# Second network: the tensor engine takes its steps in pairs, 18 products with w_in and then 24 with w_out

## The reference

```python
def _attn_ref(q, k, v, alpha):            # 4 x 8 heads, 768 steps, head size 48
    for t in range(S):
        state = alpha[:, :, t, :, None] * state + np.einsum('bhd,bhe->bhde', k[:, :, t], v[:, :, t])
        y[:, :, t] = np.einsum('bhd,bhde->bhe', q[:, :, t], state)

def _moe_ref(x, expert_emb, tau, w1, w2): # 3072 tokens, 384 features, 8 experts of 1024
    for e in range(E):
        mask = expert_idx == e
        h = np.maximum(x[mask] @ w1[e], 0.0)
        out[mask] = gate_w[mask, None] * (h @ w2[e])

def _moe2_ref(x, w_in, w_out):            # 3072 tokens, 384 -> 2048 -> 384
    h = x @ w_in
    g = np.maximum(0.01 * h, h)
    return (g @ w_out).astype(np.float32)
```

## Time and profile before

| what | us |
|---|---|
| median of 3 runs | 819.06 |
| the three runs | 817.20, 819.06, 819.26 |
| span of the profiled execution, first to last instruction | 817.2 |
| second network, first paired place (inner of step 2) to the end | 415.0 to 817.2 |
| PE busy | 801.6 (98% of the span) |
| ACT busy, DVE busy | 346.0, 452.1 |

### The profile page before, as it was taken

One profiled execution on the slowest core, in us unless ns is written; L12 is line 12 of the kernel. 1 busy time (PEld: TensorE's weight loads), 2 busy tenths in 40 slices (PEclk: granted clock), 3 DMA queues, 4 the chain that ended last, 5 costly groups with the idle time before them and its releaser, 6 DMA issues.

```text
span 817.2 us, 17577 instructions
## 1 busy us (share of the span) xinstructions
PE 801.6 (98%) x5259; PEld 719.7 (88%) x5260; DVE 452.1 (55%) x705; ACT 346.0 (42%) x643; POOL 209.0 (26%) x278
## 2 busy tenths in 40 slices
PE   7899999999999999999999999999999999999998
PEld 7788887889989989999889988889998888998987
DVE  7899987686577476566565334433433533433332
ACT  3455554565446256444443333332333333334223
POOL 6567632223343343341241021003003001001000
PEclk9999999999999999999999999999999999999999
DMA  9988762777887887897741110201201001000001
GB/s 222 256 250 248 219 225 85 265 231 278 301 290 250 283 271 225 291 312 228 201 45 21 20 39 1 40 1 39 39 0 39 0 0 39 1 1 20 20 1 39
DMA packets 64130, 108.98 MB, mean 133 GB/s; under 512 B 24199, under 2 KB 45747, under 8 KB 64080
## 3 DMA queue, kind: packets, MB, share of 16 engines
q1 hardware_dynamic: 54896, 93.47, 37.7%
q0 software_dynamic: 5888, 14.85, 5.8%
q10 hardware_dynamic: 3296, 0.06, 0.2%
HBM read 78.89 MB, written 30.85 MB: 134 GB/s over the span
## 4 chain that ended last, share of the span: by engine, by line
PE 90%; DVE 3%; DMA 3%; issue 2%; POOL 1%; ACT 0%; DVEq 0%; ACTq 0%; SPq 0%; POOLq 0%
PE bank L1772 25%; PE bank L1721 24%; PE bank L1694 15%; PE bank L1674 14%; DMA qkas<-qka 2%; PE bank L1516 2%; PE bank L1556 2%; PE bank L1533 2%; PE bank L1564 1%; PE bank L1650 1%; PE bank L1522 1%; PE bank L1576 1%; POOL kt L675 1%; DVE decay L1073 0%; DMA xg<-x_rows,slot_src 0%
## 5 line engine op out<-in xcount | busy, mean ns | idle before, releaser
L1721 PE MATMUL bank<-yT,wts 128*128 128x512 f32 x864 | 217.5, 395 | 0.3 <-DVE yT L1306 0.3
L1772 PE MATMUL bank<-wts,gs 128*128 128x384 f32 x1152 | 215.5, 335 | 0.4 <-ACT os L1023 0.2
L1772 PEld LDWEIGHTS bank<-wts,gs 128*128 128x128 f32 x1152 | 202.0, 188 | 10.9 <-issue 2.0
L1721 PEld LDWEIGHTS bank<-yT,wts 128*128 128x128 f32 x864 | 160.6, 188 | 31.4 <-DVE yT L1306 1.0
L1302 DVE TENSOR_TENSOR g<-bank,small 128x512 f32<-128x512 f32 x96 | 66.4, 691 | 173.9 <-ACT small L929 163.8
L929 ACT ACTIVATE small<-bank 128x512 f32<-128x512 f32 x96 | 57.6, 600 | 184.8 <-PE bank L1721 170.3
L1674 PE MATMUL bank<-wts,gxT 128*128 (+1 forms) x549 | 133.5, 396 | 0.2
L1674 PEld LDWEIGHTS bank<-wts,gxT 128*128 128x128 f32 x549 | 100.8, 188 | 20.8 <-issue 0.8
L1483 DVE TENSOR_TENSOR gs<-g,gs 128x512 fp32r<-128x512 f32 x96 | 66.5, 693 | 66.8 <-ACT gs L1034 61.5
L1034 ACT ACTIVATE gs<-g 128x512 fp32r<-128x512 f32 x96 | 60.8, 633 | 78.0 <-DVE g L1302 71.3
L774 POOL DMA_INDIRECT out<-os,tokens x20 | 19.7, 986 | 288.1 <-ACT os L1023 283.5
(11 more groups left out here) (179 smaller groups left out, 768.4 us busy)
## 6 DMA issues: line engine op xcount, KB each, us to landing
raw<-weights SPq DMA_DIRECT2D x60, 512.0 KB
hidden_rows<-hs SPq DMA_DIRECT2D x29, 512.0 KB
hds<-hidden_rows SPq DMA_DIRECT2D x29, 512.0 KB
qkas<-qka SPq DMA_DIRECT2D x20, 675.5 KB, 5.1
vs<-v SPq DMA_DIRECT2D x24, 192.0 KB, 3.8
x_rows<-xs SPq DMA_DIRECT2D x24, 192.0 KB, 3.7
yl<-y_rows SPq DMA_DIRECT2D x20, 192.0 KB
qkas<-qka SPq DMA_DIRECT2D x4, 227.5 KB, 6.4
```

The lines of the kernel that those rows point to most:

```text
L1721: m = pe.matmul(gps[f % 2][:, :], wts[:, 0, w_part, n:n + P], yT[:, 1 - u, y_part, k], start=(k == 0 and (w_part, y_part) == (0, 0)), stop ...
L1772: m = pe.matmul(ops[tt], gs[:, f % 4, g_part, tt * P:(tt + 1) * P], wts[:, 1, w_part, f * D:(f + 1) * D], start=(f == 0 and (g_part, w_par ...
```

## The change

Only PE's list is changed. Before, inner and outward alternate step by step. Now the loop takes two steps at once: inner of the next two steps (pair + 2 and pair + 3, at the end of a group steps 0 and 1 of the next), then outward of the two steps of this pair. The set of products, waits and signals is the same, and the lists of the other engines are the same.

```diff
-                    for f in range(FT):
-                        if f + 2 < FT:
-                            inner(t, u, f + 2)
-                        elif not end:
-                            inner(t + 1, 1 - u, f + 2 - FT)
-                        if not (end and f >= FT - 2):
-                            outward(t, u, f)
+                    for pair in range(0, FT, 2):
+                        for f in (pair + 2, pair + 3):
+                            if f < FT:
+                                inner(t, u, f)
+                            elif not end:
+                                inner(t + 1, 1 - u, f - FT)
+                        for f in (pair, pair + 1):
+                            if not (end and f >= FT - 2):
+                                outward(t, u, f)
```

## The result

Over 22 runs of each, side by side, the changed kernel took 816.10 us in the median (813.94 to 818.22) and the kernel before 818.16 us (815.38 to 819.41). The ratio is 0.9976, with a 95% interval of 0.9968 to 0.9984: 2.0 us less, 1.3 to 2.6. The difference is clear of the scatter, and smaller than the 0.3% that the prediction took as the limit of telling a change. The profiled execution of the changed kernel has a span of 813.8 us.

What follows compares the result with a forecast made beforehand. PE was taken as the bound, busy 801.6 of 817.2 us, so only waits could go: -1.70 at group starts plus 0.34 at the loop's start, -1.36 from 819.06, giving 817.7 us, range 814.4 to 819.8.

Steps and rivals of the forecast that it cites:

- Part 1: Five group starts: two inner runs, 4.20 us, hide ACT's four copies of about 2 us, so all waiting goes, -1.70 us.
- Rival C: Group starts: something else holds ACT back, the copies stay uncovered and the 1.70 us remain, 819.4 us; chance 0.06.
- Part 2: Loop's start: inner of step 3 waits for DVE's g of step 1, 0.54 us over instead of 0.20, +0.34 us.
- Part 3: The other 46 pairs: banks, remainders and buffers are ready in time, so no wait arises, 0.
- Part 4: Rate of the products: inner and outward keep their pace in longer runs, so fewer switches gain 0.
- Rival A: Pairs' products: longer runs are faster, reaching the experts' pace, 3.3 us more gone, 814.4 us; chance 0.13.
- Part 5: End of the loop: the last remainder was already hidden behind outward work and is now behind more, 0.
- Rival B: Second inner run of each pair: its load's wait for g_done costs 0.13 us a pair, 6.1 us, 823.8 us; chance 0.04.
- The clock: Whole kernel: PE's clock is granted in full in every slice, 2.4 GHz, so there is no clock to win.

Runs made afterwards that it cites:

- e11: The changed kernel itself, unaltered, measured once more in the same job as its relatives: 816.80 us, ratio 0.9989 to the kernel before.
- e1: The changed kernel with the first pair of each group taken step by step again: 818.14 us, ratio 1.0008 to the kernel before.
- e2: Only the first two steps of each group taken as a pair, all others singly as in the kernel before: 816.11 us, ratio 0.9985.
- e3: The kernel before with each of 20 ACT copies of finished tiles made twice: 830.60 us, ratio 1.0149.
- e4: The changed kernel with each of 20 ACT copies of finished tiles made twice: 817.19 us, ratio 0.9984 to the kernel before.
- e10: The kernel before, step by step, with DVE taking two of ACT's four copies of finished tiles: 816.48 us, ratio 0.9988.
- e9: The kernel before, step by step, with only PE's loop over groups written out: 817.38 us, ratio 0.9995.

## Why the prediction was right

It said 817.7 us, 1.36 less than before; measured are 816.1, 2.0 less (1.3 to 2.6), and, in the job of e11, 0.9 less (2.1 less to 0.4 more). The loop in the trace lost 1.40 us. Of the 1.6 us between 817.7 and 816.1, 0.9 lies in the starting value: it was the median of three executions, 819.06, where 22 gave 818.16.

- **Part 1, group starts: -1.70.** Measured 1.71, all of it, with 1.8 us to spare in place of "2 us". e1 and e2 show that these starts and the loop's start are the effect but for 0.1 us, e3, e4 and e10 that at the group starts it is the copies against the cover: longer copies cost 1.88 us each time where the cover is one run, and shorter ones gain without pairs. Rival C is excluded. What the prediction did not tell apart is the start of group 2: there the copies alone don't explain its 0.48 us, since with shorter copies 0.37 stayed (e10) and without the branch 0.34 (e9). The sum held because it took each start whole, and the longer cover hides both.
- **Part 2, the loop's start: +0.34.** 0.53 over against 0.20 is 0.33. Reading the time at which g ends from the old trace (417.47) worked because nothing ahead of it moved. The split of the 0.54 was right too: 0.42 of waiting and 0.11 for the slow start, for 0.41 and 0.13. The cause that it gave for the 0.20 of before was not: it put them down to DVE's late remainder, but e9, with the remainder as late and no branch, is 0.01 over. The number came out all the same, since it was read from start to start, and the changed order hides the branch as it would hide the remainder.
- **Part 3, no new wait in the other pairs.** No pair after the first departs from 8.36 us.
- **Part 4, the pace: 0.** 4.20 and 4.16 us. Rival A falls by the changed kernel's own trace. The argument that the run of 9 shows no slow beginning held; which property of the operands sets the pace was not found.
- **Part 5, the end: 0.** Nearly: the last remainder was not quite hidden before. It ended at 810.67, and the products of step 95 that needed it lost 0.03 us, which are gone.
- **Rival B**, a dent in front of the second inner run: none, beyond the first pair. The 64-entry window that the page "TensorE: Matmul & The Clock Gate" of the Trainium skill tells of, in Step-by-step, fits: the rows of 18 are unbroken, the tenth product starting 231 ns after the ninth (482.276 to 482.507), like its neighbours. The 50 to 100 ns for a semaphore read, from the Trainium skill's page "Advanced Engine Details and Errata", Network/Comms, do not appear on PE's path there.
- **The clock.** "Granted in full in every slice" reads the row of nines too strictly: both profiles have a stretch of half clock in the attention stage. In the loop it was full before and after, so nothing in the sum hangs on it.

The measured 2.0 us are 0.6 more than the loop explains. The median of 22 runs allows 1.40, and the job of e11 gives 0.9, so I take no further gain as shown. The profiled spans differ by 3.4 us, 2.0 of which arose ahead of the loop (it starts at 415.01 and 412.99), where both programs are the same; the profiles of the variants that leave that part alone start the loop anywhere from 411.9 to 414.8 us. Most of that arises in the attention stage: the first product of the experts starts at 138.42 before, at 136.09 in the changed kernel, and between 134.7 and 137.0 in those variants. Part of the scatter goes with the granted clock: of the kernel before in the job of e9 to e11, 8 executions with a mean granted clock of 1.000 took 817.0 us on average, 14 with 0.998 took 818.0, and 5 with 0.996 took 819.4. A single span therefore says nothing on a change of this size, while the loop repeated to 0.01 us in e11.

## What to carry to other kernels

An order that looks as if it saved switches may only lengthen the cover of one wait: look for the steps that take longer than the others, sum up what they are over, and ask how much work stands between the producer and the one who waits. Where the longer cover is needed only at a few places, pairing only there does nearly all of it (e2), and shortening what is waited for gives nearly as much (e10). At the very start, where the bank comes free late, the early request costs more than it gives. What looks like a wait for a late engine can be a branch on the waiting engine: compare the time at which the data were ready with the time at which the load began. When the scatter of whole runs is larger than the effect, time the stretch that the change touches, from start to start.

## What the runs showed of the hardware

- In e3 PE stood still for 1.88 to 2.10 us at five places, with the same work around each, and at three of them the granted clock then went from full, 2.4 GHz, to half, 1.2 GHz, for 3.4 us. An outward run took up to 3.44 us instead of the 2.2 that it takes after a wait at full clock. A wait that is 9.4 us by its own length cost 14.1 us in that trace. The waits of 0.15 to 0.37 us in the kernel before never did this.
- The pace of a product depends on more than its width: 512 wide it is 227 ns at the end of the experts' runs of 18 and 233 ns in the second network, there in runs of 9 and of 18 alike. Moving a tile by 32 or 64 bytes changes the pattern of starts within a run, at the same mean within 0.3%.
- Products of two kinds switch without a loss that shows: the changed kernel has 94 switches fewer, and e1, which has 82 fewer, gained 0.09 us in the loop.
- A compare-and-branch between a wait and the load costs PE time where no cover is left. On line 1789 it took 0.22 us at the loop's start and 0.18 at the start of group 2. From the moment when the data were ready, the load started 0.31 us later with it and 0.06 without at the loop's start (e9), and 0.27 (551.45 to 551.72) with it at group 2, where group 1 without it shows 0.04.
